# Running the first three tiles of the second MoE layer in straight line beside the first layer's last row and the second layer's tables

## What is computed

```
x    = depthwise causal convolution of x, 7 taps, softmaxed weights, 8 heads of 24 channels
# layer 1: only tokens with x @ w_skip > 0; the others pass unchanged
e    = argmax(x @ w_gate);  g = softmax(x @ w_gate)[e]
x    = x + g * (relu(x @ w1[e]) @ w2[e])
# layer 2: all tokens
xn   = x / |x|;  logits = xn @ normalized(expert_emb).T / tau
e    = argmax(logits);  g = softmax(logits)[e]
out  = g * (relu(x @ w1[e]) @ w2[e])
```

## Time and profile before

| | us |
|---|---|
| median of 3 runs (1260.19 to 1262.38) | 1260.75 |
| the profiled execution, timed | 1261.57 |
| its span | 1260.0 |
| TensorE busy (share of the span) | 1110.7 (88%) |
| VectorE busy | 747.9 (59%) |
| ScalarE busy | 552.9 (44%) |
| POOL busy | 436.8 (35%) |
| TensorE's mean granted clock | 0.949 |

### The profile page before, as it was taken

The page is one execution under the profiler, slowest core; times in us unless marked ns, Lnnn a source line. Parts: engine busy times, 40 slices in busy tenths (PEclk is TensorE's granted clock), DMA queues, the critical chain, the costliest instruction groups (busy, mean ns, idle before and its releaser), DMA issues.

```text
span 1260.0 us, 28656 instructions
## 1 busy us (share of the span) xinstructions
PE 1110.7 (88%) x8244; PEld 1062.5 (84%) x8245; DVE 747.9 (59%) x2132; ACT 552.9 (44%) x1487; POOL 436.8 (35%) x562
## 2 busy tenths in 40 slices
PE   4998950899999999999529999999999999999996
PEld 3876740899899999999429999999999999999996
DVE  2575770687778778778605565655556556565553
ACT  2553510343334434434115554556545555555553
POOL 3177775122122122122203333333433333333332
PEclk9999955999999999999759999999999999999998
DMA  5555133522213033031133131211313113111111
GB/s 159 145 166 170 67 112 101 132 65 69 82 39 92 27 95 93 26 93 37 62 93 94 42 93 38 84 56 38 100 42 91 38 33 103 38 37 45 38 42 35
DMA packets 61937, 94.93 MB, mean 75 GB/s; under 512 B 9523, under 2 KB 48522, under 8 KB 61776
## 3 DMA queue, kind: packets, MB, share of 16 engines
q1 hardware_dynamic: 41168, 46.16, 12.8%
q0 software_dynamic: 20736, 48.34, 12.4%
HBM read 61.21 MB, written 35.63 MB: 77 GB/s over the span
## 4 chain that ended last, share of the span: by engine, by line
PE 63%; issue 11%; POOL 10%; DVE 6%; ACT 4%; DMA 2%; SPq 1%; DVEq 1%; ACTq 1%; POOLq 0%
PE ph L760 28%; PE py L777 19%; PE py L782 9%; POOL bucket_rows L945 8%; ACT w1s L330 1%; DVE w1s L338 1%; PE pt L719 1%; POOL out_rows L400 1%; PE pt L720 1%; PE ph L1159 1%; PE ph L1160 1%; ACT w2s L331 1%; DVE h_lo L565 1%; DMA bucket_rows<-xrow,idx_row 1%; POOL g_nrm L391 1%
## 5 line engine op out<-in xcount | busy, mean ns | idle before, releaser
L777 PE MATMUL py<-w2s,h_hi 128*128 128x384 f32 x1472 | 440.4, 362 | 0.0
L760 PE MATMUL ph<-xa_hi,w1s 128*128 128x256 f32 x1472 | 389.5, 286 | 24.0 <-issue 23.6
L440 ACT ACTIVATE h_hi<-ph 128x512 fp32r<-128x512 f32 x368 | 218.9, 595 | 314.8 <-PE ph L760 314.8
L782 PE MATMUL py<-w2s,h_lo 128*128 128x192 f32 x1472 | 347.4, 256 | 7.1 <-DVE h_lo L565 6.2
L565 DVE SCALAR_TENSOR_TENSOR h_lo<-ph,h_hi 128x512 fp32r<-128x512 f32 x368 | 250.9, 689 | 154.6 <-ACT h_hi L440 152.6
L760 PEld LDWEIGHTS ph<-xa_hi,w1s 128*128 128x128 f32 x1472 | 280.0, 190 | 30.3 <-issue 29.8
L760 PE MATMUL ph<-xb,w1s 128*128 128x256 f32 x1472 | 295.7, 282 | 0.0
L782 PEld LDWEIGHTS py<-w2s,h_lo 128*128 128x128 f32 x1472 | 277.5, 190 | 10.5 <-issue 10.5
L777 PEld LDWEIGHTS py<-w2s,h_hi 128*128 128x128 f32 x1472 | 270.0, 188 | 0.8 <-issue 0.6
L760 PEld LDWEIGHTS ph<-xb,w1s 128*128 128x128 f32 x1472 | 227.6, 190 | 0.0
L760 PE MATMUL ph<-xa_lo,w1s 128*128 128x256 f32 x736 | 207.9, 282 | 0.0
(11 more groups left out here) (203 smaller groups left out, 1502.6 us busy)
## 6 DMA issues: line engine op xcount, KB each, us to landing
xg<-bucket_rows POOLq DMA_DIRECT2D x96, 202.0 KB, 2.8
w2raw<-in_moe_w SPq DMA_DIRECT2D x16, 768.0 KB, 7.3
w1raw<-in_moe_w SPq DMA_DIRECT2D x16, 512.0 KB, 3.7
w1raw<-in_moe_w SPq DMA_DIRECT2D x32, 256.0 KB, 5.2
work<-in_x SPq DMA_DIRECT2D x4, 1440.0 KB, 8.3
work<-in_x SPq DMA_DIRECT2D x4, 1344.0 KB, 8.0
bucket_rows<-fill SPq DMA_DIRECT2D x18, 202.0 KB, 2.3
out_rows<-yrow,idx_out POOLq DMA_INDIRECT x118, 2.4
```

The costliest lines, as they stand in the source:

```text
L440: act.activation(h_hi[:, 2 * q:2 * q + 2, :], ph[q][:, :].rearrange("p (c t) -> p c t", c=2), ACT.Relu).then_inc(L["h_high"], 1)
L760: ins = pe.matmul(to, w, v[:, :], start=n == 0, stop=n == len(parts) - 1)
L777: return pe.matmul(py[s][:, 0:2 * D], h_hi[:, f, t], w2s[:, slot, f, :, :].rearrange("p c d -> p (c d)"), start=f == 0, stop=f == FC - 1)
L782: return pe.matmul(py[s][:, 0:D], h_lo[:, f, t], w2s[:, slot, f, 0, :], start=False, stop=False)
```

## The change

The loop of the second layer is left for tiles 3 and up. Tiles 0, 1 and 2 are written out in straight line on every engine, all of expert 0 in slot 0, and read rows at fixed places: the first 768 rows of bucket 8. If the first phase put fewer there, they are padded, and the later rows are placed behind the padding.

- The table of the first layer runs on into bucket 8 (8 columns of `starts` and `jumps` for 7), so its gather and its transposes for "the next tile" after the last one bring tile 0 of the second layer.
- SyncE stores three fills behind the first phase's rows of bucket 8 and loads the three early tiles to SBUF (`x_early`, in the first phase's work buffers) at the start of the first layer; POOL waits for these stores after its first two gathers. The first layer has 8 fills for 9.
- The first layer's last row is transposed and scored in early tile 0, like that of any tile, and marked after `x_low` of tile 1; its totals are counted just before its places. The fills, the row table and the tile table follow in early tile 1, the second layer's gathers and the count registers in early tiles 1 and 2.
- The weights of the second layer's expert 1 are loaded in the first layer's last expert and split in early tile 2.
- `each_pair` is as it was; tile j of the loop is now 3 + 2i + u.
- `early_dve` runs on VectorE behind the first layer's tables. `tile_first_part`, `tile_middle_part` and `tile_last_part` are the steps of the second layer's tile as before, cut in three. Of the dummy scatters with which POOL starts (six), two remain.

```diff
 def first_layer_pool(pool, last_row):
...
     gather(pool, 0, 0, 0)
     gather(pool, 0, 1, 1)
     skip, full, odd = tile_counts(pool, 0)
+    pool.wait_ge(e_pad, 16 * EARLY)
...
+def second_layer_pool(pool, full0, odd0, last_row, last_token):
+    def norms(T):
+        pool.wait_ge(*T.load)
...
+        pool.tensor_copy(idx_tok[:, T.par, :], T.x[:, :, C_ID]).then_inc(L["index"], 1)
+        pool.wait_ge(L["squares"], T.j + 1)
+        pool.tensor_tensor(g_nrm[:, :], g_sqr[:, :], half[:, :], ALU.pow) \
+            .then_inc(L["norm_root"], 1)
+    def results(T):
+        pool.wait_ge(L["tile_out"], T.j + 1)
+        for s in range(SUB):
+            pool.indirect_dma_start(
+                out=out, out_offset=bass.IndirectOffsetOnAxis(ap=idx_tok[:, T.par, s:s + 1], axis=0),
+                in_=y_out[T.par][:, s, :], in_offset=None,
+                bounds_check=last_token, oob_is_err=False).then_inc(L[f"scattered{T.par}"], 16)
...
+    norms(early_tile(0))
+    pool.wait_ge(before["placed"], full0 * 2 + odd0 + 2)
+    with pool.If(odd0 > 0):
+        scatter_row(pool, 0, last_row)
+    with pool.Else():
+        scatter_row(pool, 1, last_row)
+    results(early_tile(0))
+    norms(early_tile(1))
...
+    pool.wait_ge(L["rows_known"], 1)
+    pool.wait_ge(L["filled"], 16 * FILLS[1])
+    gather(pool, 1, EARLY, 0)
+    gather(pool, 1, EARLY + 1, 1)
+    pool.wait_ge(L["tiles_known"], 1)
+    skip, full, odd = tile_counts(pool, 1)
+    results(early_tile(1))
+    for t in range(2, EARLY):
+        norms(early_tile(t))
+        results(early_tile(t))
...
+def second_layer_act(act, full0, odd0):
+    def tile_first_part(T):
+        h_high(act, 1, T.j, 0)
...
+        ins.then_inc(L["squares"], 1)
+        h_high(act, 1, T.j, 1)
+    def tile_middle_part(T):
+        h_high(act, 1, T.j, 2)
+        act.wait_ge(L["gate_bias"], T.j + 1)
...
+        h_high(act, 1, T.j, 3)
+        x_high(act, 1, T.j + 1)
...
+    T = early_tile(0)
+    tile_first_part(T)
+    y_high(act, full0 * 2 + odd0)
+    tile_middle_part(T)
+    tile_last_part(T)
+    T = early_tile(1)
...
+    T = early_tile(2)
+    tile_first_part(T)
+    tile_middle_part(T)
+    act.wait_ge(w_raw, (E + 2) * (16 * NW))
+    split_high(act, 1)
+    act.wait_ge(L["tiles_known"], 1)
+    skip, full, odd = tile_counts(act, 1)
+    tile_last_part(T)
...
+def early_dve(dve):
+    step = Chain(dve, e_chain)
+    first = s_cnt[:, E:E + 1]
+    step.did(dve.tensor_tensor(lack[:, 0:1], first, bucket_at[:, E:E + 1], ALU.add))
+    step.step(dve.tensor_scalar(lack[:, 1:2], first, -1.0, float(EARLY * TILE), ALU.mult, ALU.add))
+    dve.tensor_scalar(early_at[:, :], iota_row[:, 0:EARLY], float(TILE), lack[:, 0:1], ALU.mult, ALU.add) \
+        .then_inc(e_known, 1)
+    step.step(dve.tensor_scalar(lack_of[:, :], lack[:, 1:2], 0.0, below[:, 0:1], ALU.max, ALU.add))
+    step.step(dve.tensor_scalar(share[:, :], lack_of[:, :], P.bit_length() - 1, None, ALU.logical_shift_right))
+    step.step(dve.tensor_tensor(run2[:, 0, SUB:SUB + 1], run2[:, 0, SUB:SUB + 1], share[:, :], ALU.add))
...
+def second_layer_dve(dve, full0, odd0):
+    T = early_tile(0)
+    tile_first_part(T, chain)
+    y_low(dve, last)
+    tile_middle_part(T, chain)
+    with dve.If(odd0 > 0):
+        mark_row(dve, last, 1, row)
+    with dve.Else():
+        mark_row(dve, last, 0, row)
+    tile_last_part(T, chain)
...
+    with dve.If(odd0 > 0):
+        place_row(dve, last, 1, row)
...
+    with dve.Else():
+        place_row(dve, last, 0, row)
...
+    fills_dve(dve, 1, step)
+    T = early_tile(1)
+    tile_first_part(T, chain)
+    rows_dve(dve, 1, step)
+    tile_middle_part(T, chain)
+    infos_dve(dve, 1, step)
+    tile_last_part(T, chain)
+    T = early_tile(2)
+    tile_first_part(T, chain)
+    tile_middle_part(T, chain)
+    split_low1(dve, 1, E + 1)
+    tile_last_part(T, chain)
+    split_low2(dve, 1, E + 1)
...
+def second_layer_pe(pe, full0, odd0):
+    for q in range(FC // 2):
+        first_product(pe, 1, 0, q)
+        if q == 1:
+            pe.wait_ge(before["tile_out"], last + 1)
+            pe.wait_ge(before["placed"], last + 1)
...
+            with pe.If(odd0 > 0):
+                y_transposed(pe, 0)
+            with pe.Else():
+                y_transposed(pe, 1)
+    transposed(pe, 1, x_early[1], early_tile(1).load)
+    y_scores(pe, last)
+    for q in range(FC // 2):
+        second_product(pe, 1, 0, 0, q)
+        if q == 2:
+            pe.wait_ge(before["marked"], last + 1)
+            pe.matmul(pu[:, TOTALS:TOTALS + E], ones_b[:, :], run2[:, :, SUB], start=True, stop=True) \
+                .then_inc(L["counted"], 1)
+            row_counts(pe)
...
+    for t in range(1, EARLY):
+        pe.wait_ge(L["x_low"], t)
+        for q in range(FC // 2):
+            first_product(pe, 1, 0, q)
+        if t + 1 < EARLY:
+            transposed(pe, 1, x_early[t + 1], early_tile(t + 1).load)
+        else:
+            transposed(pe, 1, xg[:, 0], (L["loaded0"], 16))
+        pe.wait_ge(L["tile_out"], t)
+        for q in range(FC // 2):
+            second_product(pe, 1, t, 0, q)
+            if t + 1 == EARLY and q == 0:
+                pe.wait_ge(L["tiles_known"], 1)
+                look_ahead(EARLY)
...
 def fill_tiles(l):
...
     load_weights(sp, moe_w1, moe_w2, 1)
+    sp.wait_ge(e_known, 1)
+    for t in range(EARLY):
+        at = sp.value_load(early_at[0:1, t:t + 1], min_val=0, max_val=NB * CAP - TILE)
+        sp.dma_start(rows[bass.ds(at, TILE), :].rearrange("(p s) r -> p (s r)", s=SUB), fill[:, :]) \
+            .then_inc(e_pad, 16)
+    for k in range(XR):
+        sp.wait_ge(a_sc[k], SCAT * len(range(k, NG, XR)))
+    sp.wait_ge(e_pad, 16 * EARLY)
+    for t in range(EARLY):
+        at = E * CAP + t * TILE
+        sp.dma_start(x_early[t].rearrange("p s r -> p (s r)"),
+                     rows[at:at + TILE, :].rearrange("(p s) r -> p (s r)", s=SUB)) \
+            .then_inc(layers[1][f"early{t}"], 16)
     with sp.Fori(2, E) as e:
         sp.wait_ge(w_ready, e)
         load_weights(sp, moe_w1, moe_w2, e)
     sp.wait_ge(w_ready, E)
     load_weights(sp, moe2_w1, moe2_w2, 0)
+    sp.wait_ge(w_ready, E + 1)
+    load_weights(sp, moe2_w1, moe2_w2, 1)
     fill_tiles(1)
-    sp.wait_ge(layers[1]["x_low"], 1)
-    with sp.Fori(1, E) as e:
+    with sp.Fori(2, E) as e:
         sp.wait_ge(w_ready, e + E)
         load_weights(sp, moe2_w1, moe2_w2, e)
...
-    for done in (layers[0]["scattered0"], layers[1]["scattered0"], layers[1]["scattered1"]):
...
```

852 lines of the change are left out of this document (478 added, 374 removed).

## The result

| | before | after |
|---|---|---|
| median, us (4 runs each, in turns on one chip) | 1260.49 (1260.19 to 1262.38) | 1240.11 (1239.15 to 1243.70) |
| ratio, 95% interval | | 0.9846 [0.9830, 0.9861] |
| profiled execution, timed; span | 1261.57; 1260.0 | 1239.15; 1237.5 |
| TensorE busy; VectorE; ScalarE; POOL | 1110.7; 747.9; 552.9; 436.8 | 1109.6; 745.7; 551.9; 431.9 |
| mean granted clock | 0.949 | 0.960 |

The change makes the kernel 20.4 us faster by the medians. The forecast was 15.7 us (1260.75 to 1245, range 1236 to 1255). The engines do the same work; what shrank is the hole between the layers.

The account below looks back on a forecast made before the run. The second layer was taken as TensorE bound, with a hole before it. Tile 4 starting at t = 67.6 instead of 85.7 saves 18.1 us, less 2 for clock: 16.1 off 1260.75 gives 1245, range 1236 to 1255.

Parts of the forecast that it names:

- early tile 0: First straight-line tile of the second layer: TensorE waits 3.2 us for the last row's marking and ends at t = 14.6.
- early tile 1: Second straight-line tile: TensorE waits 3.0 us for a low part of h behind POOL's scatters, results and root; ends t = 28.0.
- early tile 2: Third straight-line tile: gather lands at 33.3, root done at 37.5, TensorE waits about 3 us and ends at t = 41.5.
- tile 3: First tile of the second layer's loop: 9.75 us plus 3.0 for the low clock, starting at t = 54.8.
- clock in the early tiles: Waits of 3 us may lower TensorE's clock in the three early tiles: 2 us taken, bounds 0 and 6.
- The head: TensorE's walk over skipped rounds before the second layer's loop: two code fetches, second 6 us; walk 14.4, bounds 8.6 and 17.4.
- rival 2: Second layer's loop head is cheap, one fetch or none: walk 4.6 to 8.6 us, time 1235 to 1240; chance 0.16.
- the prediction's own signs: Right if an "issue" wait of 10 to 14 us precedes the loop; wrong if the first layer ends later than 612.3.
- rival 4: At the loop's head every skipping pass pays a 4.01 us fetch: walk 33 us, time 1263.3; chance 0.03.
- The waits in the early tiles: TensorE waits 3.2 us for the marking in tile 0 and about 3 us for low parts in tiles 1 and 2.
- The first layer: Added copy, VectorE operations, stores and loads before the hole are covered by existing waits: cost taken as 0.
- both do the same: From the start of the second layer's tile 4 on, the kernels before and after take equal time.

Follow-up runs that it names:

- Experiment 1: Kernel before, with the load of the second layer's expert 1 weights issued before the fills, 20 us ahead of the head: 1313.83 against 1315.51, ratio 0.9992.
- experiment 10: 128 semaphore increments put into TensorE's stream ahead of the first layer, in the kernel before (1252.17) and in the changed kernel (1242.22), one run each.
- Experiment 6: Changed kernel, with VectorE marking the first layer's last row ahead of the first early tile's middle part: 1297.34 against the changed kernel's 1296.36 beside it.
- Experiment 4: Changed kernel, with POOL making the root of early tiles 1 and 2 before the previous tile's results: 1291.95, ratio 0.9816 to the kernel before.
- experiments 2 and 3: Loop over pairs does full rounds first, skipped rounds last: in the kernel before 1300.67, ratio 0.9869; in the changed kernel 1279.44, ratio 0.9723, again 1225.47, ratio 0.9718.

## Why the prediction was right, and where it was off

The direction, the range and the mechanism of the gain held: work that stood between the layers now runs beside tiles, and the time is 5 us below the 1245. The price of the loop's head did not hold. Against its own steps:

| step | predicted, us | measured, us |
|---|---|---|
| early tile 0 starts | 612.3 | 614.56 |
| early tile 0 | 14.6 | 13.45 |
| early tile 1 | 13.4 | 13.84 |
| early tile 2 | 13.5 | 15.4 |
| from its last product to tile 3 | 13.3 | 6.6 |
| tile 3 | 12.75 | 11.1 |
| clock in the early tiles | 2.0 | within the above; see below |
| tile 4 starts | 681.9 | 674.95 |

**The head, the step that failed.** "I take 6, nearer to the quiet one" for a second missed fetch. There was none: the walk from TensorE's first loop instructions at 655.3 to the product at 663.85 took 8.5 us for 14.4, at the lower bound of 8.6. And 2.0 us of it were hidden behind tile 2's products, not 1.1. The 8.91 us had been put down to one fetch beside the load of weights. The instruction queue shows three packets in it, in the trace that was at hand. Experiment 1 moved the load and kept the branch; experiment 10 moved the code and lost it. So the row told mainly of where the code lay and little of a busy neighbour. This was rival 2 (chance 0.16) in its mechanism. That the time, 1240.1, still came out at the border between it and the forecast is in part luck: the head was priced 6.7 us too dear and tiles 0 and 3 together 2.8, while the late start and early tiles 1 and 2 took 4.6 us more than priced, against the 2.0 set aside for the clock. Two of the prediction's own signs had gone against it: the "issue" wait was 6.6 us for 10 to 14, and the first layer ended later than 612.3.

**The Trainium skill's rule.** In the straight early tiles three packets came and nothing waited for them, while a branch in the head waits 3.3 to 4.1 us with one packet: so far the trace agrees with "Runtime: NRT & Kernel Launch", Instruction fetch mechanics. Taken for every skipping pass it does not hold: of four passes one was long, and rival 4 with it was far off.

**The waits in the early tiles** were seen nearly in size: 2.2 us for the marking (3.2 predicted; root at 621.02, 6.5 after the tile's start for 6.7, marking done 12.1 after it for 13.0), 2.5 and 2.6 for the third low parts (3.0 each). The gather landed within 0.6 us of TensorE's want. Experiment 6 shows that VectorE's order set the first. Experiment 4 shows that POOL's root set the one in tile 2, as argued; in tile 1 the prediction had the row table run harmlessly beside the root, and it is as late as the root itself.

**The clock** was mis-sized twice, in opposite ways. In the early tiles 2.0 us was rather too little: waits of 2 to 3 us left tile 0 at 1.00 and brought tiles 1 and 2 to 0.91 and 0.86 (629 to 642 and 642 to 656 above: 0.90 and 0.87). A steady tile's 9.75 us would by the clock alone become 10.7 and 11.3 there, 2.6 us more together (an estimate), and TensorE was in fact busy for 11.3 and 12.3 us, 4.0 more. By the same estimate 1.6 of the 1.9 us by which tile 2 exceeded its row are the clock's. Behind the head, 40 products took 6.24 us and not 7.71 (4.73 at full clock): 1.5 us for the 3.0 that I took from a hole of 37 us; the hole now is 8.

**The first layer** was costed at nothing and cost 2.3 us. Its first product came 1.2 us later, 0.5 of it because the head's one long branch took 3.93 us for 3.41; its first tile took 0.9 longer, and a later tile waits 0.8 us for idx_out. I have not isolated which part does this; the first tile takes 12.5 to 13.9 us over all the profiles, with or without the change, so some of it may be scatter. Behind tile 4, "both do the same" was off by 0.9: two POOL stretches of 4.25 and 1.8 us of issue hold tile 4 at 11.1 us, where it took 9.87 before.

**What the change itself is worth.** With the code shifted in both, 14.8 us in the two layers (1005.8 to 991.0); with no walk in either, 19.1 (experiments 2 and 3). The 23.3 between the first profiles holds the long branch that a mere shift of 128 instructions removed. The rows of the kernel before alone could not tell whether the change would keep that branch: the bounds, 0.2 and 8.9, were the honest part of the step, and the 6 between them was not.

## What to carry to other kernels

A loop with a fixed number of rounds should do its work first and its skipped rounds last: a layer's walk past skipped rounds held TensorE, the bottleneck, for 3.6 to 14 us here, and an edit of a few lines removed it. When a row of sequencer time looks like a code fetch, count the packets of the instruction queue in its stretch, then shift the code and measure before pricing a change against it, because such a cost can move with any edit. And where several waits overlap, mend the largest first: orders of two other engines, worth some 3 us by the tiles before the head was mended, were worth 5 behind it, though single profiles leave open how much of that difference is scatter.

## What the runs showed of the hardware that I had not expected

- A branch of TensorE in a loop's head took 3.3 to 4.1 us where it was long and 0.07 to 0.23 where not; one long one per head in most kernels, two in the kernel before at its own place (4.01 and 8.91; 3.65 and 7.09 on another chip). VectorE, ScalarE and POOL, walking the same rounds, took 34 to 73 ns for each.
- Each of these long branches has a packet of some 16 KB of the instruction queue that began within it, the 8.91 us one three; and from 654 to 1240 in the kernel before, while the loop ran, that queue moved none.
- A branch of 7.1 us came about with no load of weights beside it; with the load it was 8.9 (single branches, two chips).
- The granted clock stayed at 1.00 through a tile with a wait of 2.2 us, and stood at 0.86 and 0.91 in the next two, with waits of 2.5 to 3.2 us each.
- Two of the chips took some 40 us or more longer for the same first phase, and one of them 6 us more for the two layers of the same kernel; a ratio to the kernel before held within 0.4% all the same.
